# One core, gated attention and two MLPs: alpha products for two units at once, earlier loads, a second bank for the first up products

## The reference

```python
for t in range(S):
    state = alpha[:, :, t, :, None] * state + np.einsum('bhd,bhe->bhde', k[:, :, t], v[:, :, t])
    y[:, :, t] = np.einsum('bhd,bhde->bhe', q[:, :, t], state)
x = y.transpose(0, 2, 1, 3).reshape(B * S, H * D)
h = x @ w_in;   x = (h / (1 + np.exp(-1.702 * h))) @ w_out
h = x @ w_in2;  out = (h - np.tanh(h)) @ w_out2
```

## Time and profile before

| | us |
|---|---|
| median of three runs | 966.66 (965.78 to 969.44) |
| profiled execution | 967.3 |
| its span | 965.5 |
| TensorE, VectorE, ScalarE, GpSimd busy | 943.8, 672.2, 376.4, 285.4 |

### The profile page before, as it was taken

One profiled execution on the slowest core, in us unless ns is written; L12 is line 12 of the kernel. 1 busy time (PEld: TensorE's weight loads), 2 busy tenths in 40 slices (PEclk: granted clock), 3 DMA queues, 4 the chain that ended last, 5 costly groups with the idle time before them and its releaser, 6 DMA issues.

```text
span 965.5 us, 23370 instructions
## 1 busy us (share of the span) xinstructions
PE 943.8 (98%) x9705; PEld 830.0 (86%) x9705; DVE 672.2 (70%) x1615; ACT 376.4 (39%) x730; POOL 285.4 (30%) x314
## 2 busy tenths in 40 slices
PE   5899999999999999999999999999999999999998
PEld 4789999999999988888888888888888888888886
DVE  7879997878888877776322544357677677776765
ACT  1352333332332332333234664244444444444442
POOL 2666665646556554444001642000000000000000
PEclk9999999999999999999999999999999999999999
DMA  7943232423323332321113322010020020100101
GB/s 156 256 89 91 49 86 51 114 49 85 80 61 83 90 69 47 104 47 25 19 58 123 98 82 90 1 37 30 1 66 2 1 66 1 40 27 1 34 1 33
DMA packets 136234, 58.94 MB, mean 61 GB/s; under 512 B 114368, under 2 KB 131520, under 8 KB 136128
## 3 DMA queue, kind: packets, MB, share of 16 engines
q1 hardware_dynamic: 133488, 55.39, 22.8%
q10 hardware_dynamic: 2640, 2.05, 0.7%
HBM read 43.26 MB, written 13.96 MB: 59 GB/s over the span
## 4 chain that ended last, share of the span: by engine, by line
PE 92%; DVE 3%; DMA 2%; SPq 1%; POOL 1%; issue 1%; ACT 0%; DVEq 0%; POOLq 0%; ACTq 0%
PE pX L840 39%; PE pZ L864 16%; PE pX L864 9%; PE pZ L908 6%; PE pZ L914 6%; PE pX L908 4%; PE pX L704 3%; PE pZ L799 2%; PE pZ L732 2%; PE pZ L690 1%; PE pZ L742 1%; DMA k<-k_t 1%; PE pX L835 1%; PE pX L718 1%; PE pZ L790 1%; DVE scores L1212 1%
## 5 line engine op out<-in xcount | busy, mean ns | idle before, releaser
L840 PE MATMUL pX<-x_hi,w_hi 128*128 128x512 f32 (+2 forms) x624 | 227.7, 365 | 0.7 <-ACT g L1050 0.7
L840 PE MATMUL pX<-x_lo,w_hi 128*128 128x512 f32 (+2 forms) x624 | 227.3, 364 | 0.0
L840 PE MATMUL pX<-x_hi,w_lo 128*128 128x512 f32 (+2 forms) x624 | 227.3, 364 | 0.0
L1228 DVE TENSOR_TENSOR g_lo<-g,g_hi 128x512 fp32r<-128x512 f32 (+2 forms) x208 | 129.3, 637 | 87.5 <-ACT g_hi L1059 87.3
L1059 ACT ACTIVATE g_hi<-g 128x512 fp32r<-128x512 f32 (+2 forms) x208 | 121.3, 583 | 89.5 <-DVE g L1308 85.9
L1050 ACT ACTIVATE g<-pX 128x512 f32<-128x512 f32 (+3 forms) x144 | 65.7, 456 | 206.4 <-PE pX L840 173.2
L1308 DVE TENSOR_TENSOR g<-pX,sg 128x512 f32<-128x512 f32 x96 | 66.3, 690 | 106.2 <-ACT sg L1052 106.2
L840 PEld LDWEIGHTS pX<-x_hi,w_hi 128*128 128x128 f32 x624 | 117.5, 188 | 18.0 <-ACT g L1050 1.1
L840 PEld LDWEIGHTS pX<-x_lo,w_hi 128*128 128x128 f32 x624 | 117.5, 188 | 16.9
L840 PEld LDWEIGHTS pX<-x_hi,w_lo 128*128 128x128 f32 x624 | 117.5, 188 | 16.8
L596 POOL TENSOR_TENSOR r<-r,alpha 112x128 f32<-112x128 f32 (+2 forms) x115 | 109.5, 968 | 18.5 <-DMA r<-q_t 14.9
(11 more groups left out here) (166 smaller groups left out, 1899.4 us busy)
## 6 DMA issues: line engine op xcount, KB each, us to landing
v<-v_l SPq DMA_DIRECT2D x96, 48.0 KB, 2.6
x_raw<-hidden SPq DMA_DIRECT2D x6, 768.0 KB, 5.7
attn_out<-y SPq DMA_DIRECT2D x92, 48.0 KB, 1.8
out_t<-o SPq DMA_DIRECT2D x10, 384.0 KB, 3.5
alpha<-a_t SPq DMA_DIRECT2D x24, 128.0 KB, 2.9
r<-q_t SPq DMA_DIRECT2D x24, 128.0 KB, 3.0
k<-k_t SPq DMA_DIRECT2D x24, 128.0 KB, 3.0
w_raw<-w_in SPq DMA_DIRECT2D x16, 192.0 KB, 2.4
```

The lines of the kernel that those rows point to most:

```text
L840: last = nc.tensor.matmul(pH(N)[:, 0:w], win(wp, f, m), XS[T % 2][xp][:, m, 0:w], start=(n == 0), stop=(n == len(terms) - 1))
L1228: nc.vector.tensor_tensor(at(GLs, N), g_raw(N), at(GHs, N).bitcast(F32), ALU.subtract).then_inc(gl_done, 1)
```

## The change

- **Alpha of two units.** AL, SF1, T4, T16, F4, F16 and T64 hold two units, `part_of(U)` is a unit's half. `product_step` works on both halves at once, for units 1 and 2, 3 and 4, ...; unit 0 is alone. `ahead` skips the even units at odd items. T64 was one tile for each parity and is now written for both units at once. Alpha of both must have landed, and GpSimd's first part waits for both too. `load_alpha` is called twice at odd U.
- **Loads.** Alpha of unit 1, q and k of unit 1 go ahead of v of unit 0; alpha of unit 2 behind it, q and k of unit 2 behind v of unit 1, ahead of the pieces of x. ScalarE issues its two weight loads once q of unit 1 has landed. The ten pieces of x are divided otherwise: SyncE issues six, ScalarE four. The quarters of the weights stand at other places.
- **First unit.** Product steps 0 to 7 run ahead of q's first multiply.
- **Banks.** Up products 1 and 3 go to O0. Up 2 to 4 wait for the GELU of N-2; down products wait for at least four GELUs, down 0 also for the states of items 0 and 1.
- **ScalarE.** y of item 0 is copied, and two pieces issued, ahead of the query copy of unit 1. Up to period 31 the query copy is in the visit's own period, behind the key copy and the GELU, and no longer in the period before.
- **Visits** 3 to 7 are a period later: 5, 9, 13, 17, 21; from 25 on as before.
- **x_low** of tile 2 is in the visit at period 25, behind `states` and ahead of `ahead`, no longer at period 29. `x_high` stays.
- One warm-up product less.

```diff
-    starts = ([0, 4, 8, 12, 16, 20, 25, 30] + ...
+    starts = ([0, 5, 9, 13, 17, 21, 25, 30] + ...
+XLOW_AT = {1: 9}
...
         def pH(N):
+            if N in (1, 3):
+                return O0
             return H0 if N < L1B * NF or N % 2 == 0 else H1
...
+        def part_of(U):
+            n = (U + 1) % 2
+            return slice(n * SL, (n + 1) * SL)
...
             def load_alpha(U):
-                if U:
-                    sp.wait_ge(t_step, (U - 1) * T_STEPS + T_AL)
-                    sp.wait_ge(q_step, (U - 1) * Q_STEPS + Q_AL)
+                if U > 1:
+                    sp.wait_ge(t_step, batch_of(U - 2) * T_STEPS + T_AL)
+                    sp.wait_ge(q_step, (U - 2) * Q_STEPS + Q_AL)
                 load_a(sp, U)
...
             load_k(sp, 0, 0)
+            load_alpha(1)
             sp.dma_start(MASK[:], masks).then_inc(mask_loaded, 16)
+            load_qk(1)
             load_v(0)
-            load_alpha(1)
-            load_qk(1)
+            load_alpha(2)
...
             load_v(1)
+            load_qk(2)
...
-                    first_inputs(sp, ((0, 0), (0, 1), (1, 0), (1, 1)))
+                    first_inputs(sp, ((0, 0), (1, 0)))
                 sp.wait_ge(y_copied, 2 * U)
                 if U == 1:
-                    first_inputs(sp, ((2, 0), (3, 0)))
+                    first_inputs(sp, ((2, 1), (3, 1)))
...
-                if U + 2 < UNITS:
-                    load_alpha(U + 2)
+                for W in (U + 2, U + 3):
+                    if U % 2 and W < UNITS:
+                        load_alpha(W)
...
-                    if N:
-                        pe.wait_ge(g_done, N)
+                    if N > 1:
+                        pe.wait_ge(g_done, N if N > 4 else N - 1)
...
-                    pe.wait_ge(g_done, N + 1)
+                    pe.wait_ge(g_done, max(4, N + 1))
...
+                if N == 0:
+                    pe.wait_ge(state_step, states_before(LEAD))
...
             plain_queries(0)
+            act.wait_ge(q_loaded[1], 32)
             load_w(act, 0)
+            copy_outputs(0)
+            act.wait_ge(y_copied, 1)
+            first_inputs(act, ((0, 1), (1, 1)))
             plain_queries(1)
-            copy_outputs(0)
             copy_outputs(1)
             act.wait_ge(y_copied, 2)
-            first_inputs(act, ((2, 1), (3, 1)))
+            first_inputs(act, ((2, 0), (3, 0)))
...
-            queries_at = {VISIT_OF[j + 1] - 1: j // 2 + 1 for j in range(LEAD, ITEMS - 2, 2)}
+            queries_at = {VISIT_OF[j + 1] - (VISIT_OF[j + 1] >= L1P): j // 2 + 1 for j in range(LEAD, ITEMS - 2, 2)}
...
             def product_step(U, s):
-                a, sf1 = ([t[:].rearrange("p (c s b) -> p c s b", s=4, b=16)[:, :, d, :] for d in range(4)]
-                          for t in (AL, SF1))
+                both = slice(part_of(U).start, part_of(batch_end(U) - 1).stop)
+                a, sf1 = ([t[:, both, d * 16:(d + 1) * 16] for d in range(4)] for t in (AL, SF1))
...
-                    mul(T64[U % 2][:], F16[:, :, 2], F16[:, :, 5])
+                    mul(T64[:, both], f16[:, :, 2], f16[:, :, 5])
...
-                for s in range(3):
+                for s in range(8):
                     product_step(0, s)
                 dve.wait_ge(q_loaded[0], 32)
                 mul(r.slot[:, :, 0:4, :], r.q, r.al)
-                product_step(0, 3)
...
-                for s in range(4, 8):
-                    product_step(0, s)
                 key_step(0, 0)
...
-                if U >= UNITS:
+                if U >= UNITS or j % 2 and U % 2 == 0:
                     return
...
                         states(j)
+                        if XLOW_AT.get(T) == f:
+                            x_low(T + 1)
                         ahead(j, 0)
...
-                if f == x_at(T) and PLAIN <= T + 1 < ALLB:
+                if f == x_at(T) and T not in XLOW_AT and PLAIN <= T + 1 < ALLB:
                     x_low(T + 1)
```

More of the change, by code:

```diff
@@ L110, in made, with batch_of, batch_end @@
     return item_of(j)[3] < CHUNKS - 1
+def batch_of(U):
+    return (U + 1) // 2
+def batch_end(U):
+    return min(2 * batch_of(U), UNITS - 1) + 1
 def keys_before(j):
@@ L129, in visits @@
 def visits():
-    starts = ([0, 4, 8, 12, 16, 20, 25, 30] + [33 + 3 * n for n in range(5)] + [49 + 3 * n for n in range(5)]
+    starts = ([0, 5, 9, 13, 17, 21, 25, 30] + [33 + 3 * n for n in range(5)] + [49 + 3 * n for n in range(5)]
               + [64 + 2 * n for n in range(29)])
@@ L243, in build @@
         V = [sb(f"v_{u}", [P, 2, QP, D], where=att) for u in U2]
-        T64 = [sb(f"t64_{u}", [PX, SL], where=att) for u in U2]
+        T64 = sb("t64", [PX, 2 * SL], where=att)
         Y = [sb(f"y_{u}", [PX, 2, QP, C], where=att) for u in U2]
[L246 to L251, removed]
+        AL = sb("alpha", [PX, 2 * SL, C], where=att)
+        SF1 = sb("sf1", [PX, 2 * SL, C], where=att)
+        T4 = sb("t4", [PX, 2 * SL, 4, 4], where=att)
+        T16 = sb("t16", [PX, 2 * SL, 4], where=att)
+        F4 = sb("f4", [PX, 2 * SL, 8, 4], where=att)
+        F16 = sb("f16", [PX, 2 * SL, 8], where=att)
         S = sb("state", [PX, 2, SL, D], where=att)
@@ L376, in load_rows @@
                 eng.dma_start(part, rows[at:at + (HS, D)[h]]).then_inc(done, 16)
+        def part_of(U):
+            n = (U + 1) % 2
+            return slice(n * SL, (n + 1) * SL)
         def load_a(eng, U, half=None):
-            load_rows(eng, AL[:].rearrange("p (s t) -> p s t", s=SL), aT, U, al_loaded, half)
+            load_rows(eng, AL[:, part_of(U), :], aT, U, al_loaded if U else al0_loaded, half)
         def load_q(eng, U, half=None):
@@ L552, in _ @@
                 if U == 1:
[L553 to L556 removed]
+                    load_w(sp, 1)
                 if U + 1 < UNITS:
@@ L959, in _ @@
             pe.wait_ge(y_copied, 1)
-            warm_up(pZ[0], 15)
+            warm_up(pZ[0], 14)
             for kind, N in PRODUCTS:
@@ L1110, in product_step @@
                 if s == 0:
-                    dve.wait_ge(al_loaded, (U + 1) * 32)
                     if U:
+                        dve.wait_ge(al_loaded, (batch_end(U) - 1) * 32)
                         dve.wait_ge(k4_ready, U)
+                    else:
+                        dve.wait_ge(al0_loaded, 32)
                     mul(sf1[1], a[2], a[3])
@@ L1128, in product_step @@
                         dve.wait_ge(k16_ready, U)
-                    mul(F4[:, :, 2:6:3, :], T4[:, :, 0:4:2, :], T4[:, :, 1:4:2, :])
+                    mul(f4[:, :, 2:6:3, :], t4[:, :, 0:4:2, :], t4[:, :, 1:4:2, :])
                 elif s == 5:
-                    copy(F4[:, :, 1:7:5, :], T4[:, :, 0:4:3, :])
+                    copy(f4[:, :, 1:7:5, :], t4[:, :, 0:4:3, :])
                 elif s == 6:
                     after(5)
-                    mul(F4[:, :, 3:5, :], F4[:, :, 2:6:3, :], T4[:, :, 2:0:-1, :])
+                    mul(f4[:, :, 3:5, :], f4[:, :, 2:6:3, :], t4[:, :, 2:0:-1, :])
                 elif s == 7:
-                    mul(T16[:], F4[:, :, 2, :], F4[:, :, 5, :])
+                    mul(t16, f4[:, :, 2, :], f4[:, :, 5, :])
                 elif s == 8:
@@ L1186, in states @@
                         nc.vector.scalar_tensor_tensor(
-                            out=S[:, (ch + 1) % 2, s, :], in0=S[:, ch % 2, s, :], scalar=T64[U % 2][:, s:s + 1],
+                            out=S[:, (ch + 1) % 2, s, :], in0=S[:, ch % 2, s, :], scalar=T64[:, part_of(U).start + s:part_of(U).start + s + 1],
                             in1=pP[:, 2 * z + q, :], op0=ALU.mult, op1=ALU.add).then_inc(state_step, 1)
```

65 lines of the change are left out of this document (33 added, 32 removed).

## The result

| | before | after |
|---|---|---|
| median, us | 967.55 (965.78 to 970.41, 12 runs) | 971.54 (969.87 to 973.74, 12 runs) |
| profiled execution | 967.3 | 972.34 |
| its span | 965.5 | 970.5 |

The ratio is 1.0043, with an interval of 1.0031 to 1.0054. The forecast was 962.3, that is 4.4 less, and the range ended at 966.5; it came 4.0 more.

A forecast was written before the change was run, and what follows sets the result against it. TensorE was taken as the bound, busy 943.8 of 965.5 us. Start gains 0.9 + 3.2 + 2.2 = 6.3, less 1.9 for x_low, gave 4.4 off 966.66: 962.3 us, range 959.3 to 966.5.

The forecast's parts named there:

- 0.9 earlier: Start-up: x lands 0.9 us earlier, so the first up product starts at 23.8; bounds 0 and 1.4.
- hide behind the warm-up: Unit 1's twelve double-width product steps take 2.6 us instead of 2.0, hidden since keys are needed only after up 0.
- The wait at period 33: New TensorE wait of 2.5 us for VectorE's scores 9, from moving x_low; 3.8 if a key step loses the port.
- the gains of the start reach the end one for one: TensorE is nearly always busy from about 56 us, so changes in the first 56 us reach the end in full.
- the distance stays: Unit 3's stores and the load hang on the visit at period 25, so x_hi ends 10.2 us after its start.
- (a): Start-up loss: first up product at 24.70 after 1.03 us waiting for x; forecast at 23.8.
- The clock: Rival: TensorE stands still at the start and its clock falls to half speed, +9.5 us, 971.8; chance 0.06.
- (b): Up products 1 to 4 start every 1.30 us, waiting for one bank; two banks give 0.67. With (c) 3.2 us.
- (c): Item 2's outputs wait 1.14 us for VectorE's scores; to be covered by 0.2. With (b) a gain of 3.2 us.
- (d): At item 5 TensorE waits 2.2 us for ScalarE's key copy; the wait goes, gain 2.2, bounds 1.5 and 2.2.
- x_low at period 25: VectorE waits for x_hi; 2.5 us wait at period 33, 0.59 wait gone; net loss 1.9, bounds 0 and 3.2.
- cost nothing itself: Visits from period 5: same count of visits and products, scores get one more period, no cost.

The follow-up runs named there:

- number 10: Kernel before with only the query copies put behind the key copies: 967.28 us against 967.09, ratio 0.9998.
- number 12: Kernel before with query copies behind key copies and low parts of w_out one per period (26 to 41): 965.48 us against 968.82, ratio 0.9972.
- number 1: Changed kernel with x_low of tile 2 back at period 29: 969.89 us, ratio 1.0010 to the kernel before.
- number 7: Number 6 with x_low of tile 2 back at period 29: 965.62 us, ratio 0.9978 to the kernel before.
- number 8: Number 7 with low parts of w_out one per period (26 to 41) and two tiles for T64: 963.28 us, ratio 0.9946 to the kernel before.
- number 5: The changed kernel run once more, unaltered, for comparison on the same chip: 972.44 us, ratio 1.0039 to the kernel before.
- number 2: Changed kernel with 24 products in the second warm-up instead of 14: 974.18 us, ratio 1.0060 to the kernel before.
- number 4: Changed kernel with GpSimd's first part of unit 1 waiting for alpha of unit 1 alone: 970.77 us, ratio 1.0020 to the kernel before.
- number 6: Number 4 with q and k of unit 2 issued behind the pieces of x: 970.65 us, ratio 1.0027 to the kernel before.
- number 3: Kernel before with only x_low of tile 2 moved to the visit at period 25: 973.53 us, ratio 1.0043.
- number 9: Kernel before with only the two banks for up 0 to 4 and the first six visits a period later: 967.10 us against 967.09, ratio 0.9999.
- Number 11: Number 8 with SyncE's loads of alpha 3 and 4 and w_in's last quarter behind q and k of unit 3: 972.48 us, ratio 1.0055 to the kernel before.

## Why the prediction was wrong

Three steps failed, with these sizes in the profile. The first up product: x's landing "0.9 earlier" was 0.65 later, since four loads that I took as covered hold SyncE's queue (1.55 us). Unit 1's products that "hide behind the warm-up" didn't hide (2.4 us). The wait at period 33: 4.24 us and not 2.5, and a lowered clock behind it that the sum left out (6.1 us from period 30 to 36 instead of 1.9). The step under all of them, that the gains of the start reach the end one for one, held here, for a reason that the prediction had only for x_low; it fails in the kernel before.

**"What the change does in the first 56 us reaches the end one for one."** Between 60 and 100 us TensorE was busy for 39.89 of 40 us, and I read that as TensorE being the bound. It was one of two: VectorE, at 36.70, had 0.3 us to spare at period 33 (my own figure: ready at 97.8, wanted at 98.09). In the kernel before the step fails: number 10 is 1.95 us ahead at period 25 and 0.06 at 33, and number 12 shows the cure. Whether it fails depends on what VectorE last stood for. The starts of two visits, in us:

| | period 25 | period 33 | between |
|---|---|---|---|
| before | 79.86 | 98.09 | 18.2 |
| number 10 | 77.91 | 98.03 | 20.1 |
| number 12 | 77.58 | 95.62 | 18.0 |
| number 1 | 81.63 | 101.74 | 20.1 |
| number 7 | 76.94 | 97.08 | 20.1 |
| number 8 | 78.39 | 96.43 | 18.0 |
| changed kernel | 78.83 | 101.19 | 22.4 |
| number 5, the same | 79.82 | 102.35 | 22.5 |
| number 2 | 77.71 | 100.01 | 22.3 |
| number 4 | 76.08 | 98.04 | 22.0 |
| number 6 | 77.12 | 98.96 | 21.8 |
| number 3 | 83.40 | 105.41 | 22.0 |

In the last six x_low is at period 25, and VectorE's chain starts again from x_hi, which hangs on that visit, as the prediction said ("the distance stays"): the distance is 21.8 to 22.5 with period 25 anywhere from 76.08 to 83.40, so a head start passes. It passes between numbers 1 and 7 too, where VectorE last stood for TensorE. In number 10 VectorE last stood for a load, and nothing of the 1.95 us passes. The prediction had not looked at this; it used the 0.3 for the price of x_low's move and did not hold it against the gains.

**(a) First up product at 23.8: it came at 25.35.** I priced the shorter work on VectorE and took SyncE's four loads ahead of x, 2.6 us by my own count and 4.4 measured (15.25 to 19.65), as covered. Number 4 alone leaves up 0 at 25.00; moving them behind x as well brings it to 24.06, 23.45 and 23.84 in numbers 6 to 8: within the bounds of the forecast. The wait for alpha of unit 2 on GpSimd, with ScalarE's copies queued behind it, I had in the diff and costed nowhere.

**The clock.** "My times leave 0.9" was wrong because x was late: the stand was 2.95 us, and up 0 to the end of visit 2 ran at the lower clock. The rival had its place and its condition right, and its price of 9.5 us too high: 2.4 us to up 1, and by number 2, where up 0 to up 1 still takes 6.4 us at the full clock, nearly all of that covers the late keys. "Slower" had a chance of 0.06, all of it for the clock. What made the kernel slower was the late keys and the visit at period 33 together, and the prediction gave these no chance of doing so.

**(b), (c) The two banks.** The pace was right: 24 matmuls in 3.24 us, 2.94 where the clock is full. The wait for scores ahead of item 3 went in the changed kernel. In the changed kernel up 1 to visit 3 took 4.51 us with one pair more done, 5.98 before: 2.8 of the 3.2 us came. Alone (number 9) it is 1.3 at visit 3, since VectorE's scores set that visit, and nil at the end.

**Products of two units, hidden behind the warm-up.** I wanted the keys by 26; from 19.36 on products and keys took 9.5 us, to 28.9. Number 4 tells two parts apart: about 2.4 us from GpSimd's work falling into the same time, the rest in single steps that are held up: there a COPY of 112x32 took 1.27 us beside GpSimd (at 22.81), the one of 112x128 before it 0.21. The trace of the kernel before had the warning: unit 1's twelve steps took 4.6 us there (20.52 to 25.10), where I put 2.0, and one copy of them 1.26. The copies in number 4 and in the kernel before:

```profile
22.81 1.27 DVE L1137 COPY f<-t 112x32 f32<-112x32 f32 x1
```

```profile
23.23 1.26 DVE L1105 COPY f<-t 112x16 f32<-112x16 f32 x1
```

**(d) The key copy.** Right: the wait of 2.2 us is gone in all kernels with that edit. Its worth at the end is nil without relief for VectorE.

**x_low at period 25.** The mechanism was right: the place (period 33), VectorE idle before x_lo (1.53 us, by ScalarE's x_hi), the wait of 0.59 at period 36 gone. The size was not: 4.24 instead of 2.5. My sum of 20.7 us came to 22.3: x_hi 0.35 later, scores 0.2 longer, and the two key steps 2.3 us instead of 1.2, because the second took 1.76 us and not 0.69. And the stand itself brought the clock down (visit 33's first products 0.68 us instead of 0.45), which took another 2.6 us up to period 36 that the sum didn't have at all (1.2 to 2.2 in numbers 2 to 6). Number 3 measured the whole at 4 to 5 us, on a kernel without the rest of the change.

The 1.76 us (1.75 in number 3) are what the row of GpSimd had warned of from the other side: VectorE lost this time. The Trainium skill (SBUF — State Buffer, Who interferes with whom) has it so, that whoever issues first blocks the other for its whole instruction. By it I had put 1.3 us more on the key steps, and they took 1.1 more; with it the wait was to be 3.8 us, and 4.24 was measured. I had it in hand and kept the 2.5. One instruction is not the most that is lost, though: see the last point of this text.

**Visits from period 5 "cost nothing itself".** They cost nothing in the changed kernel, where x_hi sets x_lo. But a later visit hands VectorE its work later: 0.8 us of it was missing at period 33 in number 9, and the period's 1.35 us are most of the 1.9 in number 7.

Added up on the profile: predicted 6.3 from the start, less 1.55 (up 0), 2.4 (clock and keys up to up 1), 0.4 (up 1 to visit 3) and 0.73 (issue), leaves 1.2; 1.0 was measured. Then 4.1 at period 33 and 2.0 behind it instead of 1.9 together.

## What to carry to other kernels

Before a gain at the start is carried to the end, look on every engine that the bounding one waits for at its last idle time ahead of the next deadline. If that idle time is for the bounding engine, a head start passes. If it is for a load or a third engine, the head start is worth no more than the slack at the deadline. Here that slack was 0.3 us on VectorE, and giving sixteen operations of 0.5 us one period each brought some 2 us more, both in the old kernel (numbers 10 and 12) and in the changed one (7 and 8). When operands of two units are batched, give each load its own semaphore, or the first consumer waits for the last load; and what is loaded ahead goes behind the transfers on which the path hangs.

## What was not expected of the hardware

- **Stands and the clock.** The granted clock fell behind the stands of 2.87 to 4.07 us at up 0 (changed kernel, numbers 4 and 1), 2.76 at item 5 (number 3) and 3.73 to 4.41 at period 33 (numbers 2 to 6; 4.24 in the changed kernel, 0.91 in the stretch 100 to 140). It held after 0.68 and 1.03 us. For stands between these both happened. It held behind 1.63 us (up 6 in number 6 took 0.94 us), 2.2 at item 5 in the kernel before and 2.32 in number 2. It fell behind 1.58 in number 8, where up 6 took 1.24 us and the clock from 40 to 42 us read 0.50, and behind 2.13 in number 9:

```profile
38.14 1.24 PE L859 MATMUL pX<-x_raw,w_raw 128*128 128x128 f32 x6 [1.58 <-issue]
```

- **A stand that nothing releases.** Ahead of up 6, or near it, TensorE stood for 0.7 to 2.4 us in the changed kernel and in numbers 1, 5 to 8 and 11. It is not in the kernel before, nor in numbers 3, 10 and 12, which keep its start, nor in number 4; numbers 2 and 9 have 0.4 and 0.5 us of it. The profile calls it "issue". It costs number 8 some 1.6 us and a lowered clock behind it. Number 11 excludes five of SyncE's loads and speaks against full DMA engines; the cause stays open.
- **The same program starts differently.** Up 0 came at 25.35 in one execution of the changed kernel and at 24.64 in another, and the four up products took 3.24 and 4.57 us. At period 25 the first was 1.0 us ahead of the kernel before, the other level with it: one profile's 1.0 is no more exact than that. The clock differs as well, and the time with it: of the 85 executions of the kernel before beside these runs, the 25 at a granted clock of 1.000 span 964.2 to 966.5 us, the 16 at 0.996 span 966.2 to 970.3.
- **GpSimd waits for a whole run of VectorE's instructions.** In the kernel before and in numbers 1, 7, 9, 10 and 12 GpSimd's 112x512 multiply starts beside VectorE's run of w_lo and x_lo and ends 1.2 us after the scores behind x_lo begin: at 95.30, after 94.07, and in number 10 at 95.24, after 94.02, though it had started at 89.98. Undisturbed it takes 1.28 us. So it looks as if it got nothing done until the run of eight w_lo and x_lo was over, and it took up to 5.28 us in all. In the changed kernel it had started ahead of the key step, and the key step was the one that waited.
